# First batch's down projection in rounded high and low parts, two heads later

## The chip, the cores and the metric

One NeuronCore of one Trainium2 chip. The metric is the device time of one execution in microseconds; the median of several executions counts. Before: 638.56 us, median of 3 runs (638.52 to 638.67).

## The reference, cut to what matters

```python
# q, k, v: (2, 8, 768, 64); sliding window of 128 keys plus 4 sink keys; softmax; times v
x = attention(q, k, v)                      # (2, 768, 512)
# mixer 1: U (768, 32), V (32, 768), w_ch1 (512, 2048), w_ch2 (2048, 512)
h = x.transpose(0, 2, 1) @ U @ V            # x.T @ U is the "down projection" of this case
u = x + h.transpose(0, 2, 1)
x = u + np.maximum(u @ w_ch1, 0.0) @ w_ch2
# mixer 2: the same form with w_tok1 (768, 256), a relu, w_tok2, and 1536 hidden channels
```

All in fp32.

## The kernel before

TensorE is faster on a rounded fp32 format (float32r) than on plain fp32. To keep fp32 precision, an operand is cut in a high part (rounded by ScalarE's Copy, L858, L942) and a low part (the operand less its high part, by GpSimd, L837, L543, or VectorE, L1148). A product is then three rounded matmuls (high·high, high·low, low·high), or two where one side carries both of its parts in its columns.

`plan` is one list of steps. Every engine goes through it in order and issues its own instructions for each step, with semaphore waits between engines. An engine's queue is strictly in order: what stands behind a waiting instruction waits as well. The order of the plan is therefore the order of the work.

**Attention, first batch.** Tiles T = 0 to 5 of 128 queries, 8 heads each; a head step has the number u = 8T + h. `attention(b)` (L64) builds for each u a unit: scores(u) (three rounded matmuls, L1364), the product with v of step u-4 (`pv`, L1394), and the transposes of the probabilities of u-2 (`probsT`, L1374). For scores(u) VectorE adds the mask and takes the maximum (L1093, "masked" here), ScalarE takes exp (L908), GpSimd copies the sink probabilities (L791). The transposes land in one of two PSUM banks in turn (banks 4 and 0, which qT, kT and sinksT use as well) and are copied to SBUF by ScalarE for odd u (L917), by VectorE for even u (L1112). In between lie, for the next tile, the transposes of q and k (`qT` at head 0, `kT` at head 2, L1341; copies on ScalarE, L868 and L877), and their high and low parts: VectorE's casts (L1048, L1071), GpSimd's subtractions q_lo (L532) and k_lo in two halves (L543; `ksplit` at head 4, `ksplit_odd` at head 6). At head 4 of tile T+1 comes `sinkpv` of tile T (L1403), after which VectorE writes x_nat, the attention's output for tile T (L1122, L1125). Three single pieces also lie on VectorE: a part of v_sink (L1040, ahead of scores 9 and 14), and V4's cast and subtraction (L1131, L1134) behind x_nat of tile 2.

**Down projection, first batch.** `("down", 1, 0, T-1)` stands at the end of head 5 of tile T (T = 1 to 5); the one of tile 5 stands by itself after the attention. It is one plain fp32 matmul (L1422), which the profile shows as two: stationary U3_sb (three copies of U side by side, 96 columns), moving x_nat (512 columns), accumulated over the six tiles in bank 3. ScalarE and VectorE then make of the three row groups the high and low parts in `low4` (L932, L1138), and the up projection multiplies 96 rows of low4 with 96 rows of V4_sb (L1472, L1538).

**Down projection, second batch.** It uses the rounded format already: `usplit` (L933, L1139) makes U4, whose 128 columns per tile are three copies of U's high part and one of its low part; `x1split` (L937, L1145) makes the high and low parts of x; two rounded matmuls per tile (L1415).

After 80 us the mixers run, with the second batch's attention laid between the matmuls of the first batch's mixer.

The lines around the old down projection:

```python
            if b == 0 and h == 5 and T > 0:
                now.append(("down", 1, b, T - 1))
...
                        pe.wait_ge(x_ready, t + 1)
                        last = mm(m_tile(use)[0:3 * RANK, :], U3_sb[:, t, :], x_nat[:, b, t, :],
                                  start=(t == 0), stop=(t == NQ - 1))
```

Of the kernel before, what the change touches and what calls it, by code (L numbers as in the profile page):

```python
# [5 lines left out]
def attention_then_two_mixers(  # L6
# [26 lines left out]
    f32 = mybir.dt.float32  # L33
# [5 lines left out]
    DM = H * D  # L39
# [24 lines left out]
    def attention(b):  # L64

        lo, hi = b * NQ * H, (b + 1) * NQ * H
        units, late = [], []
        LAG_T, LAG_V = LAGS[b]
        for u in range(lo, hi + LAG_V):
            T, h = divmod(u, H)  # L70
            now, scores, probsT, pv = [], [], [], []
            if u == 0:
                now += [("qT", T), ("kT", T), ("qsplit", T), ("ksplit", T)]
            sinks_after = u - (LAG_T if b else LAG_V)
            sinks = [("sinksT", sinks_after // H)] if lo <= sinks_after < hi and sinks_after % H == H - 1 else []
            if b == 0:
                now, sinks = now + sinks, []
            if u < hi and T + 1 < NTILES:
                if h == 0:
                    now.append(("qT", T + 1))  # L80
                if h == (2, 3)[b]:
                    now += [("kT", T + 1), ("qsplit", T + 1)]
                if h == (4, 5)[b]:
                    now.append(("ksplit", T + 1))
                if h == (6, 7)[b]:
                    now.append(("ksplit_odd", T + 1))
            if u < hi:
                scores.append(("scores", u))
            if lo <= u - LAG_T < hi:
                probsT.append(("probsT", u - LAG_T))  # L90
            if lo <= u - LAG_V:
                pv.append(("pv", u - LAG_V))
            sinkpv = [("sinkpv", (u - LAG_V) // H)] if lo <= u - LAG_V and (u - LAG_V) % H == H - 1 else []
            if b == 0 and u < hi + LAG_V - 1:
                pv, late = late + pv, sinkpv
            else:
                pv = pv + late + sinkpv
            now += scores + pv + probsT + sinks
            if u == hi and b == 0:
                now.append(("ksinks", NQ))  # L100
            if b == 0 and h == 5 and T > 0:
                now.append(("down", 1, b, T - 1))
            units.append(now)
        return units
# [191 lines left out]
    with ExitStack() as ctx:  # L296
        def sb(name, shape, dt=f32):
            return ctx.enter_context(nc.sbuf_tensor(name, shape, dt))

        def sem(name):  # L300
            return ctx.enter_context(nc.semaphore(name))
# [26 lines left out]
        with ExitStack() as early:  # L328
# [22 lines left out]
            probs = eb("probs", [P, 4, NK])  # L351
            probs_T = eb("probs_T", [P, 2, 2 * P])

        b_hi = sb("b_hi", [P, 7, 2, HALF], f32r)
        b_lo = sb("b_lo", [P, 7, 2, HALF], f32r)
        x2_hi, x2_lo = (part[:, 5:7].rearrange("p a k t -> p (a k t)")[:, 0:2 * DM].rearrange("p (t d) -> p t d", t=2)
# [57 lines left out]
        probs_ready = sem("probs_ready")  # L414
        psink_ready = sem("psink_ready")
        tp_ready = sem("tp_ready")
        u_high = sem("u_high")
        u_split = sem("u_split")
        x1_high = sem("x1_high")
# [423 lines left out]
        def _(act):  # L843
# [5 lines left out]
            for s in plan:  # L849
# [78 lines left out]
                    act.wait_ge(probs_ready, H * (T + 1))  # L928
                    nc.scalar.add(sums_eps[:, T % 2, :], sums[:, T % 2, :], 1.0e-9).then_inc(eps_added, 1)
                elif s[0] == "down" and s[1] == 1 and s[3] == NQ - 1:  # L930
                    rows = (4 if s[2] else 3) * RANK
                    high_of((s[:3], 0), rows, low4[0:rows, :], ACT.Copy)  # L932
                elif s[0] == "usplit":  # L933
                    act.wait_ge(x_ready, NTILES)
                    for part, ts in zip(U4_parts, (slice(0, KD), slice(KD, NQ))):
# [80 lines left out]
        def _(dve):  # L1016
# [15 lines left out]
            for s in plan:  # L1032
# [103 lines left out]
                elif s[0] == "down" and s[1] == 1 and s[3] == NQ - 1:  # L1136
                    rows = slice(RANK, 2 * RANK)
                    low_of((s[:3], 0), rows, low4[rows, :], low4[rows, :])  # L1138
                elif s[0] == "usplit":  # L1139
                    dve.wait_ge(U_loaded, 48)  # L1140
                    for n, (part, ts) in enumerate(zip(U4_parts, (slice(0, KD), slice(KD, NQ)))):
# [137 lines left out]
        def _(pe):  # L1279
# [52 lines left out]
            for s in plan:  # L1332
# [72 lines left out]
                elif s[0] == "down" and s[1] == 1:  # L1405
                    _, layer, b, t = s
                    use = (s[:3], 0)
                    if t == 0:
                        pe.wait_ge(U_loaded, 48)
                        m_free(use)  # L1410
                    if b:
                        pe.wait_ge(u_split, 2)
                        pe.wait_ge(x1_split, t + 1)
                        for n, x in enumerate((x2_hi, x2_lo)):
                            last = mm(m_tile(use)[:, :], U4_parts[t // KD][:, t % KD, :], x[:, t % 2, :],  # L1415
                                      start=(t == 0 and n == 0), stop=(t == NQ - 1 and n == 1),
                                      skip_group_check=True)
                        if t < NQ - 1:
                            last.then_inc(down1_done, 1)
                    else:  # L1420
                        pe.wait_ge(x_ready, t + 1)
                        last = mm(m_tile(use)[0:3 * RANK, :], U3_sb[:, t, :], x_nat[:, b, t, :],  # L1422
                                  start=(t == 0), stop=(t == NQ - 1), skip_group_check=True)
# [24 lines left out]
                elif s[0] == "up":  # L1448
# [19 lines left out]
                    for d in parts_of(s):  # L1468
                        rows = slice(d * P, (d + 1) * P)
                        if layer == 1:  # L1470
                            ranks = slice(0, (4 if b else 3) * RANK)
                            last = mm(m_tile((s[:4], d))[:, 0:HALF], low4[ranks, rows], V4_sb[ranks, cols],  # L1472
                                      start=False, stop=True, skip_group_check=True)
                        else:
# [44 lines left out]
                elif s[0] == "mm2":  # L1519
# [10 lines left out]
                    for i in range(TPH):  # L1530
# [3 lines left out]
                        if begins(s):  # L1534
                            m_free(use)
                            if layer == 1:
                                ranks = slice(0, (4 if b else 3) * RANK)
                                mm(m_tile(use)[:, :], V4_sb[ranks, here], low4[ranks, :], start=True, stop=False,  # L1538
                                   skip_group_check=True)
                            else:  # L1540
# [39 lines left out]
```

## Time and profile before

| | before |
|---|---|
| median of 3 runs | 638.56 us |
| profiled execution: time, span | 638.47 us, 636.4 us |
| TensorE busy (matmuls; weight loads) | 619.0 us (97%); 556.3 us (87%) |
| VectorE, ScalarE, GpSimd busy | 360.0, 326.5, 396.8 us |
| granted TensorE clock, mean | 1.00 |
| L1422, the fp32 down projection | 12 records, 24.3 to 76.8 us from the start |
| loads of U | 3, issued from 8.6 to 9.8 us, 2.8 us to landing |
| L1472 (up projection, 96 and 128 rows) | 16 records, 0.336, 0.422 and 0.442 us (min, median, max) |
| first mm1 of the first batch's mixer (L1515) | starts at 80.55 us |

All times inside the execution are microseconds from the start of the span. "Busy" of TensorE is modelled, since matmuls overlap; the distance from one start to the next says more. An engine's "idle before" names what it waited for, as inferred from semaphores.

### The profile page before, as it was taken

What the parts mean: (1) busy time and instruction counts of PE and PEld (TensorE: products, weight loads), DVE (VectorE), ACT (ScalarE), POOL (GpSimd) and SP (SyncE); (2) the same over time, 40 slices, a digit from 0 to 9 for tenths busy, and PEclk for the clock granted to TensorE, in tenths of its full rate; (3) what the DMA queues carried; (4) which work ended last, traced back from release to release, by engine and by line L of the source; (5) the groups of instructions that cost most, each with busy time, mean ns of one, the idle gap of its engine ahead of it and who ended that gap; (6) DMA issues with size and microseconds to landing.
All of it is one profiled execution on the core that took longest, in us unless ns stands there. A gap on an engine that the chain in (4) does not pass through costs nothing.

```text
span 636.4 us, 10351 instructions
## 1 busy us (share of the span) xinstructions
PE 619.0 (97%) x3466; PEld 556.3 (87%) x3466; DVE 360.0 (57%) x757; ACT 326.5 (51%) x728; POOL 396.8 (62%) x420
## 2 busy tenths in 40 slices
PE   8899889999999998999999999999999999999997
PEld 7889778989989997999999988899998888999986
DVE  7776664563654546775665741396577226665411
ACT  5657755545545465754454444545444447454321
POOL 8644656878878684557565654576657446667252
PEclk9999999999999999999999999999999999999999
DMA  8444243543343434322323332432333353421252
GB/s 175 108 95 117 71 127 86 132 117 100 92 125 100 134 88 128 92 91 75 110 82 108 91 109 75 120 110 87 95 90 114 91 145 97 148 83 34 51 155 76
DMA packets 88467, 65.59 MB, mean 103 GB/s; under 512 B 43040, under 2 KB 72480, under 8 KB 88416
## 3 DMA queue, kind: packets, MB, share of 16 engines
q1 hardware_dynamic: 88416, 64.95, 36.6%
q8 instruction: 28, 0.46, 0.3%
q14 instruction: 23, 0.19, 0.1%
HBM read 61.52 MB, written 3.15 MB: 102 GB/s over the span
## 4 chain that ended last, share of the span: by engine, by line
PE 85%; DVE 8%; issue 3%; ACT 2%; POOL 1%; DMA 0%; DVEq 0%; ACTq 0%; POOLq 0%
PE bank L1550 33%; PE bank L1321 23%; PE bank L1515 9%; PE bank L1394 4%; PE bank L1364 3%; PE bank L1479 3%; PE bank L1441 3%; PE bank L1374 2%; PE bank L1341 1%; DVE b_lo L1194 1%; PE bank L1455 1%; DVE masked L1093 1%; PE bank L1422 1%; PE bank L1542 1%; DVE b_lo L1148 1%
## 5 line engine op out<-in xcount | busy, mean ns | idle before, releaser
L837 POOL TENSOR_TENSOR w_lo<-w_raw,w_hi 128x512 fp32r<-128x512 f32 (+1 forms) x158 | 208.7, 1328 | 140.8 <-ACT w_hi L858 140.7
L858 ACT ACTIVATE w_hi<-w_raw 128x512 fp32r<-128x512 f32 (+1 forms) x158 | 96.7, 618 | 54.2 <-PE bank L1550 36.2
L1550 PE MATMUL bank<-w_hi,hid_hi 128*128 128x512 f32 x216 | 86.7, 401 | 0.3 <-DVE hid_lo L1025 0.3
L908 ACT ACTIVATE probs<-masked,neg_max 128x264 f32<-128x264 f32 x96 | 49.5, 516 | 70.7 <-DVE neg_max L1093 70.3
L1550 PE MATMUL bank<-w_hi,hid_lo 128*128 128x512 f32 x216 | 85.0, 394 | 0.0
L1550 PE MATMUL bank<-w_lo,hid_hi 128*128 128x512 f32 x216 | 84.9, 393 | 0.0
L1550 PE MATMUL bank<-w_hi,y_hid 128*128 128x512 f32 x216 | 71.0, 394 | 0.2
L1093 DVE CUSTOM_DVE_ANT_0 masked<-bank,masks 128x264 f32<-128x264 f32 x96 | 41.1, 429 | 26.8 <-PE bank L1364 23.3
L1394 PE MATMUL bank<-v_nat,probs_T 128*128 128x64 f32 x352 | 50.7, 263 | 1.8 <-DVE probs_T L1112 1.2
L1394 PEld LDWEIGHTS bank<-v_nat,probs_T 128*128 128x128 f32 x352 | 48.0, 190 | 3.8 <-ACT probs_T L917 1.7
L1550 PEld LDWEIGHTS bank<-w_hi,y_hid 128*128 128x128 f32 x216 | 40.5, 188 | 9.5 <-POOL w_lo L837 1.5
L1550 PEld LDWEIGHTS bank<-w_hi,hid_lo 128*128 128x128 f32 x216 | 40.5, 188 | 8.9
L1321 PE MATMUL bank<-b_hi,a_hi_even 128*128 128x384 f32 x140 | 47.1, 336 | 0.1
L1550 PEld LDWEIGHTS bank<-w_hi,hid_hi 128*128 128x128 f32 x216 | 40.7, 188 | 7.4 <-issue 0.7
L1321 PE MATMUL bank<-b_hi,a_lo_even 128*128 128x384 f32 x140 | 47.0, 336 | 0.0
L1321 PE MATMUL bank<-b_hi,a_lo_odd 128*128 128x384 f32 x140 | 47.0, 336 | 0.0
L1321 PE MATMUL bank<-b_hi,a_hi_odd 128*128 128x384 f32 x140 | 46.9, 335 | 0.0
L1321 PE MATMUL bank<-b_lo,a_hi_odd 128*128 128x384 f32 x140 | 46.9, 335 | 0.0
L1321 PE MATMUL bank<-b_lo,a_hi_even 128*128 128x384 f32 x140 | 46.9, 335 | 0.0
L1550 PEld LDWEIGHTS bank<-w_lo,hid_hi 128*128 128x128 f32 x216 | 40.6, 188 | 6.7
L1515 PE MATMUL bank<-uT_hi,w_hi 128*128 128x384 f32 x128 | 45.3, 354 | 0.4 <-DVE uT_lo L1028 0.4
L1025 DVE SCALAR_TENSOR_TENSOR hid_lo<-bank,hid_hi 128x384 fp32r<-128x384 f32 x32 | 17.8, 556 | 48.4 <-ACT hid_hi L846 48.4
(173 smaller groups left out, 1528.7 us busy)
## 6 DMA issues: line engine op xcount, KB each, us to landing
w_raw<-in_moe_w_ch_dram SPq DMA_DIRECT2D x144, 256.0 KB, 2.7
w_raw<-in_moe_w_ch_dram SPq DMA_DIRECT2D x20, 512.0 KB, 3.5
q_nat<-in_q_dram SPq DMA_DIRECT2D x12, 256.0 KB, 3.0
k_nat<-in_k_dram SPq DMA_DIRECT2D x12, 256.0 KB, 3.5
v_nat<-in_v_dram SPq DMA_DIRECT2D x12, 256.0 KB, 3.5
out_dram<-o_stage SPq DMA_DIRECT2D x11, 256.0 KB, 3.4
w_raw<-in_moe_w_tok_dram SPq DMA_DIRECT2D x6, 256.0 KB, 2.6
w_raw<-in_moe_w_tok_dram SPq DMA_DIRECT2D x8, 192.0 KB, 2.4
```

The lines of the kernel that those rows point to most:

```text
L837: nc.gpsimd.tensor_tensor(w_lo[:, split % NW, 0:n], w_raw[:, split % NR, 0:n], w_hi[:, split % NW, 0:n].bitcast(f32), ALU.subtract) \
L858: nc.scalar.activation(w_hi[:, split % NW, 0:n], w_raw[:, split % NR, 0:n], ACT.Copy) \
L908: nc.scalar.activation(probs[:, u % 4, :], masked[:, u % 3, :], ACT.Exp, bias=neg_max[:, u % (2 * H):u % (2 * H) + 1], scale=-1.0, accum_o ...
L1025: nc.vector.scalar_tensor_tensor(out=dst, in0=src, scalar=0.0, in1=hi.bitcast(f32), op0=ALU.max, op1=ALU.subtract).then_inc(m_drained, 1)
L1093: nc.vector.tensor_tensor_reduce(out=masked[:, u % 3, :], in0=s_slots(u)[0][:, 0:NK], in1=masks[:, mask_of(T), :], scale=1.0, scalar=3.0e3 ...
L1321: last = mm(bank[:, 0:HALF], w[at % 2][:, a, k, :], u[:, b_part, k, :], start=(first and n == 0), stop=(n == 5), skip_group_check=True)
L1364: last = mm(bank[:, 0:NK], queries, keys(ks, T, h // 2, h % 2), start=(n == 0), stop=(n == len(passes) - 1))
L1394: last = mm(o_bank(T)[:, h * D:(h + 1) * D], probs_T[:, u % 2, j * P:(j + 1) * P], v_nat[:, tile % 3, h * D:(h + 1) * D], start=(h == 0 an ...
L1441: last = mm(m_tile(use)[:, :], w[:, slot, cols], x[:, t % 2, :], start=(t == 0 and n == 0), stop=(t == NQ - 1 and n == 2), skip_group_chec ...
L1479: last = mm(m_tile((s[:4], d))[:, 0:HALF], tok[:, g, rows], w[:, slot, 0:HALF], start=False, stop=(g == KG - 1 and n == 2), skip_group_che ...
L1515: last = mm(m_tile(use)[:, 0:HALF], w[:, slot, rows], u[:, kk, cols], start=(n == 0), stop=(n == 3 * KD - 1))
L1550: last = mm(m_tile(use)[:, :], stationary, w[:, slot, :], start=False, stop=(final and n == 2), skip_group_check=True)
```

## The change

In the first batch the down projections of tiles 0 to 4 are made as in the second batch: a step `u0split` (end of head 1 of tile 1) makes U4 for all six tiles in an unused part of uT_lo, 128 x 576 columns on ScalarE and 128 x 192 on VectorE. A step `x0split` (end of head 5 of tile T) makes the high and low parts of x of tile T-1, 128 x 512 each, in two slots in uT_hi and uT_lo. The down projection itself moves from the end of head 5 to the end of head 7 and waits for both steps. Tile 5 stays one fp32 matmul in its old place, into 96 of the 128 rows. low4 and V4_sb are used with 128 rows in both batches.

```diff
--- before.py
+++ after.py
@@ -98,7 +98,11 @@
             now += scores + pv + probsT + sinks
             if u == hi and b == 0:
                 now.append(("ksinks", NQ))
+            if u == H + 1:
+                now.append(("u0split",))
             if b == 0 and h == 5 and T > 0:
+                now.append(("x0split", T - 1))
+            if b == 0 and h == 7 and T > 0:
                 now.append(("down", 1, b, T - 1))
             units.append(now)
         return units
@@ -350,6 +354,9 @@
             masked = eb("masked", [P, 3, NK])
             probs = eb("probs", [P, 4, NK])
             probs_T = eb("probs_T", [P, 2, 2 * P])
+
+        x0_hi, x0_lo = (part[:, 0:2, 0:DM] for part in (uT_hi, uT_lo))
+        U4_first = uT_lo[:, KD - 1, :].rearrange("p (t r) -> p t r", t=NQ)
 
         b_hi = sb("b_hi", [P, 7, 2, HALF], f32r)
         b_lo = sb("b_lo", [P, 7, 2, HALF], f32r)
@@ -414,6 +421,11 @@
         probs_ready = sem("probs_ready")
         psink_ready = sem("psink_ready")
         tp_ready = sem("tp_ready")
+        u0_high = sem("u0_high")
+        u0_split = sem("u0_split")
+        x0_high = sem("x0_high")
+        x0_split = sem("x0_split")
+        down0_done = sem("down0_done")
         u_high = sem("u_high")
         u_split = sem("u_split")
         x1_high = sem("x1_high")
@@ -928,8 +940,16 @@
                     act.wait_ge(probs_ready, H * (T + 1))
                     nc.scalar.add(sums_eps[:, T % 2, :], sums[:, T % 2, :], 1.0e-9).then_inc(eps_added, 1)
                 elif s[0] == "down" and s[1] == 1 and s[3] == NQ - 1:
-                    rows = (4 if s[2] else 3) * RANK
-                    high_of((s[:3], 0), rows, low4[0:rows, :], ACT.Copy)
+                    high_of((s[:3], 0), 4 * RANK, low4[:, :], ACT.Copy)
+                elif s[0] == "u0split":
+                    act.wait_ge(U_loaded, 48)
+                    nc.scalar.activation(U4_first[:, :, 0:3 * RANK], U3_sb[:, :, :], ACT.Copy).then_inc(u0_high, 1)
+                elif s[0] == "x0split":
+                    t = s[1]
+                    act.wait_ge(x_ready, t + 1)
+                    if t >= 2:
+                        act.wait_ge(down0_done, t - 1)
+                    nc.scalar.activation(x0_hi[:, t % 2, :], x_nat[:, 0, t, :], ACT.Copy).then_inc(x0_high, 1)
                 elif s[0] == "usplit":
                     act.wait_ge(x_ready, NTILES)
                     for part, ts in zip(U4_parts, (slice(0, KD), slice(KD, NQ))):
@@ -1136,6 +1156,16 @@
                 elif s[0] == "down" and s[1] == 1 and s[3] == NQ - 1:
                     rows = slice(RANK, 2 * RANK)
                     low_of((s[:3], 0), rows, low4[rows, :], low4[rows, :])
+                elif s[0] == "u0split":
+                    dve.wait_ge(U_loaded, 48)
+                    dve.wait_ge(u0_high, 1)
+                    nc.vector.tensor_tensor(U4_first[:, :, 3 * RANK:4 * RANK], U3_sb[:, :, 0:RANK],
+                                            U4_first[:, :, 0:RANK].bitcast(f32), ALU.subtract).then_inc(u0_split, 1)
+                elif s[0] == "x0split":
+                    t = s[1]
+                    dve.wait_ge(x0_high, t + 1)
+                    nc.vector.tensor_tensor(x0_lo[:, t % 2, :], x_nat[:, 0, t, :], x0_hi[:, t % 2, :].bitcast(f32),
+                                            ALU.subtract).then_inc(x0_split, 1)
                 elif s[0] == "usplit":
                     dve.wait_ge(U_loaded, 48)
                     for n, (part, ts) in enumerate(zip(U4_parts, (slice(0, KD), slice(KD, NQ)))):
@@ -1408,7 +1438,14 @@
                     if t == 0:
                         pe.wait_ge(U_loaded, 48)
                         m_free(use)
-                    if b:
+                    if b == 0 and t < NQ - 1:
+                        pe.wait_ge(u0_split, 1)
+                        pe.wait_ge(x0_split, t + 1)
+                        for n, x in enumerate((x0_hi, x0_lo)):
+                            last = mm(m_tile(use)[:, :], U4_first[:, t, :], x[:, t % 2, :],
+                                      start=(t == 0 and n == 0), stop=False, skip_group_check=True)
+                        last.then_inc(down0_done, 1)
+                    elif b:
                         pe.wait_ge(u_split, 2)
                         pe.wait_ge(x1_split, t + 1)
                         for n, x in enumerate((x2_hi, x2_lo)):
@@ -1468,7 +1505,7 @@
                     for d in parts_of(s):
                         rows = slice(d * P, (d + 1) * P)
                         if layer == 1:
-                            ranks = slice(0, (4 if b else 3) * RANK)
+                            ranks = slice(0, 4 * RANK)
                             last = mm(m_tile((s[:4], d))[:, 0:HALF], low4[ranks, rows], V4_sb[ranks, cols],
                                       start=False, stop=True, skip_group_check=True)
                         else:
@@ -1534,7 +1571,7 @@
                         if begins(s):
                             m_free(use)
                             if layer == 1:
-                                ranks = slice(0, (4 if b else 3) * RANK)
+                                ranks = slice(0, 4 * RANK)
                                 mm(m_tile(use)[:, :], V4_sb[ranks, here], low4[ranks, :], start=True, stop=False,
                                    skip_group_check=True)
                             else:
```

## Rows read from the trace of the kernel before

**Rows 1.** Windows: stretch, its length, busy us (instructions) of PE, PEld, DVE, ACT, POOL, clock, DMA.
```profile
14.00:20.00 6.00, 4.62 (x34) 4.03 (x34) 4.87 (x20) 4.28 (x17) 3.82 (x8) 1.00 0.69 157
...
29.00:39.00 10.00, 9.86 (x82) 8.89 (x81) 6.71 (x25) 6.84 (x24) 5.33 (x11) 1.00 0.35 80
```

**Rows 2.** Line L1422: min/median/max ns of one, first and last start; idle before it.
```profile
L1422 PE MATMUL bank<-x_nat,U_sb x12: 592/616/670, 24.3 to 76.8; 128*96 128x512 f32 x12
...
  DVE x_nat L1125: 3.9, 8
```

**Rows 3.** Timeline, tile 2, heads 4 to 7: start us, duration us, engine, line.
```profile
33.63 0.29 PE L1364 MATMUL bank<-k_lo,q_hi 128*128 128x264 f32 x1
...
34.98 0.42 DVE L1093 CUSTOM_DVE_ANT_0 masked<-bank,masks 128x264 f32<-128x264 f32 x1
...
35.45 0.52 ACT L908 ACTIVATE probs<-masked,neg_max 128x264 f32<-128x264 f32 x1 [0.91 <-DVE neg_max L1093]
...
35.85 0.29 PE L1364 MATMUL bank<-k_lo,q_hi 128*128 128x264 f32 x1
...
35.97 0.36 ACT L917 ACTIVATE probs_T<-bank 128x256 f32<-128x256 f32 x1
...
36.29 0.43 DVE L1093 CUSTOM_DVE_ANT_0 masked<-bank,masks 128x264 f32<-128x264 f32 x1 [0.88 <-PE bank L1364]
36.45 1.28 POOL L543 TENSOR_TENSOR k_lo<-uT_full,k_hi 64x512 fp32r<-64x512 f32 x1
...
36.84 0.28 PE L1364 MATMUL bank<-k_lo,q_hi 128*128 128x264 f32 x1
...
38.89 0.39 PE L1374 MATMUL bank<-ident,probs 128*128 128x128 f32 x2
```

**Rows 4.** Timeline of TensorE at the second batch's down projection, a rounded pair.
```profile
243.46 0.39 PE L1415 MATMUL bank<-b_hi 128*128 128x512 f32 x1
...
243.91 0.39 PE L1415 MATMUL bank<-b_hi 128*128 128x512 f32 x1
```

**Rows 5.** Lines of the second batch's splits: min/median/max ns of one.
```profile
L942 ACT ACTIVATE b_hi<-x_nat x6: 614/625/633, 236.9 to 244.7; 128x512 fp32r<-128x512 f32 x6
...
L1148 DVE TENSOR_TENSOR b_lo<-x_nat,b_hi x6: 676/688/1776, 238.3 to 246.2; 128x512 fp32r<-128x512 f32 x6
...
L936 ACT ACTIVATE b_hi<-U_sb x1: 514/514/514, 236.2 to 236.2; 128x384 fp32r<-128x384 f32 x1
L936 ACT ACTIVATE b_lo<-U_sb x1: 353/353/353, 236.6 to 236.6; 128x192 fp32r<-128x192 f32 x1
...
L1143 DVE TENSOR_TENSOR b_lo<-U_sb,b_lo x1: 209/209/209, 238.2 to 238.2; 128x64 fp32r<-128x64 f32 x1
```

**Rows 6.** A GpSimd subtraction in the timeline, and line L1083, which began beside it.
```profile
72.67 1.27 POOL L837 TENSOR_TENSOR w_lo<-w_raw,w_hi 128x512 fp32r<-128x512 f32 x1 [0.62 <-ACT w_hi L858]
...
L1083 DVE TENSOR_TENSOR k_lo<-uT_full,k_hi x2: 206/752/1298, 72.7 to 74.0; 64x48 fp32r<-64x48 f32 x2
```

**Rows 7.** Timeline, tile 3, the same places: k_lo, and transposes of step 30.
```profile
48.80 1.28 POOL L543 TENSOR_TENSOR k_lo<-uT_full,k_hi 64x512 fp32r<-64x512 f32 x1
...
50.65 0.39 PE L1374 MATMUL bank<-ident,probs 128*128 128x128 f32 x2
```

**Rows 8.** Timeline, tile 1 (u0split's place, then x0split's), and tile 5.
```profile
19.96 0.58 ACT L877 ACTIVATE uT_full<-bank 128x512 f32<-128x512 f32 x1
...
20.44 0.51 ACT L908 ACTIVATE probs<-masked,neg_max 128x264 f32<-128x264 f32 x1
...
26.25 1.28 POOL L543 TENSOR_TENSOR k_lo<-uT_full,k_hi 64x512 fp32r<-64x512 f32 x1
...
28.39 0.39 PE L1374 MATMUL bank<-ident,probs 128*128 128x128 f32 x2
...
69.88 1.29 POOL L543 TENSOR_TENSOR k_lo<-uT_full,k_hi 64x512 fp32r<-64x512 f32 x1
...
72.12 0.66 PE L1394 MATMUL bank<-v_nat,probs_T 128*128 128x64 f32 x4 [0.21 <-ACT probs_T L917]
```

## Prediction, made before the changed kernel was run

> **What bounds the kernel now.** I read the busy shares and the windows first, then the costliest lines, then the waits, and last the timeline around each place that is edited. Over the whole span TensorE is busy 97%, and from 80 us on, in the mixers, nearly without a gap. The change lies before that, in the first batch's attention (about 9 to 77 us). There the windows show TensorE 9.86 of 10 us busy beside VectorE 6.71 and ScalarE 6.84 [rows 1]. That looks like a stage paced by TensorE, and by it the change would be a gain. The timeline says less. A head step u (scores, probs·V of u-4, transposes of u-2) goes round a ring of three engines: scores on TensorE, masked on VectorE (L1093), exp on ScalarE (L908), transposes on TensorE, their copy on ScalarE (odd u) or VectorE (even u), product on TensorE. Each engine takes its part in the order of the plan. The ring has some 1.5 us of slack, and the down projection sits where it is smallest: in head 5 of each query tile VectorE has just made x_nat (0.69 us), so its copy of step u-3's transposes and masked(u) are late, and TensorE waits 3.9 us in all for x_nat before L1422 [rows 2]. From one key-low scores matmul to the next the step with the down projection takes 33.63 to 35.85 = 2.22 us, the ordinary one after it 35.85 to 36.84 = 0.99 [rows 3]: the fp32 down costs 1.23 us, some 0.93 of it work (two passes of the array of 0.616 us as recorded, overlapping; the next instruction is through 0.93 us after) and 0.3 waiting.
>
> **TensorE's part: less work.** Five times an fp32 pair (0.93 us) becomes two rounded matmuls of 128x512. The second batch already does the same; a pair there takes 243.46 to 243.91 = 0.45 us [rows 4]. That is 0.48 us less, 2.4 us over five tiles. Moved from head 5 to head 7 it no longer waits for x_nat. The last tile stays fp32 and stays where it was (0). The matmuls with V4 and low4 take 128 rows in place of 96, and a matmul's time goes by its columns: in both forms L1472 is 0.34 to 0.44 us, so 0. ScalarE's reading of the down bank has 128 partitions in place of 96, 512 columns as before: 0.
>
> **What is added.** ScalarE: x high, 128x512, five times 0.625 us; U high, 576 columns, once. Its two neighbours are 0.514 us for 384 columns and 0.353 for 192, so 0.84 ns a column and 0.675 us. VectorE: x low, 0.688 us when undisturbed, five times; U low, 192 columns, between 0.209 (64 columns) and 0.688 (512), near the small one: 0.35 us [rows 5]. Together 3.8 us on each, in 70 us of which each is 60 to 70% busy. By shares both fit. They are charged by place.
>
> **x0split, head 5 of query tile 2 (u = 21).** It stands behind the end of step 21, so ScalarE does exp(21), the copy of step 19's transposes, and only then x high; VectorE does masked(21) and then *stands* before x low until x high is there, with masked(22), the copy of step 20 and masked(23) queued behind it. In the old timeline exp(21) starts at 35.45 and the copy at 35.97 [rows 3]; neither depends on the removed matmul, since both hang on VectorE's x_nat and masked(21) at 34.98. So x high runs about 36.3 to 36.9. VectorE, free from 35.4, starts x low near 36.9, where before masked(22) had started at 36.29.
> Then GpSimd. At 36.45 it starts its k_lo subtraction (1.28 us, to 37.73), and that start hangs on exp(21) and does not move. x low reads two SBUF operands, as k_lo does. Where such a VectorE operation meets a GpSimd one in this trace, it ends with it: L1083, 64x48, took 1298 ns beside a GpSimd subtraction from 72.67 to 73.94 and 206 ns after it [rows 6]; L1148's longest of six is 1776 ns against a median of 688 [rows 5]. I therefore let x low end at 37.73 + 0.56 = 38.29 (its own columns, about 0.68 less the start-up that passes while it waits), not at 37.6.
> The Trainium skill has this as a rule ("SBUF — State Buffer", "SBUF: two separate sides"): the port pair shared by VectorE and GpSimd is an exclusive lock, taken for a whole instruction by a VectorE op with two SBUF inputs or by a GpSimd op. By it x low waits in all five tiles; the trace agrees at L1083. By the same skill's "VectorE: DVE Perf Modes" alone, which puts an fp32 two-input operation of 512 columns at 691 ns, it would be through in 0.69 us: that is the second case below.
> From there the chain is: masked(22) 0.36, copy of 20's transposes 0.33 (both start to start, since neighbouring VectorE rows overlap by some 0.08), masked(23) 0.43, exp(23) 0.52, ScalarE's copy of 21's transposes 0.36 (its PSUM bank is the one that the transposes of 22 need), and two hops between engines of 0.04, less the 0.08 by which masked(22) overlaps x low: 2.0 us. Transposes(22) start at 40.29, where they stood at 38.89 [rows 3]: **+1.4 us**. The down pair itself waits for x low (38.3, TensorE arrives at 36.9) and lies inside this; so the 0.48 us saved per pair, and the removed wait, buy an earlier arrival at a longer wait. Afterwards the ring runs as before and the next x_nat is as late as the ring, so nothing is given back before the next tile.
>
> **The other tiles, by the same steps:** end of k_lo, + 0.56, + 2.0, against the old start of the matching TensorE work.
> Tile 4 repeats tile 2: +1.4.
> Tile 3: k_lo 48.80 + 1.28; 52.64 against 50.65 [rows 7]: +2.0. Here VectorE's V4 cast and subtraction had delayed everything already, and the old down projection lay hidden behind them; taking it away gains nothing here.
> Tile 1: k_lo 26.25 + 1.28; here the v_sink subtraction (L1040, as many columns as x low: 0.6 us start to start) also queues behind x low; 30.7 against 28.39 is 2.3 [rows 8]; GpSimd's earlier work might start it 0.3 earlier: I take +2.1.
> Tile 5: k_lo 69.88 + 1.29; 73.73 against 72.12 [rows 8]: +1.6, passed on through scores(48) to the last x_nat and so to the first up projection.
>
> **u0split, head 1 of tile 1.** ScalarE's 0.675 us goes ahead of the k copy that started at 19.96; VectorE stands for it, does U low, and only then q_hi's cast and masked(10), which it had long done. 19.96 + 0.67 + 0.04 + 0.27 + 0.34 + 0.43 + 0.04 = 21.75 for exp(10), against 20.44 [rows 8]: +1.3, of which about **+1.2** reaches x_nat of tile 0. The chip shows in this stretch no slack on TensorE that would help, since it waits there for these very engines. Bounds: 0.6 (ScalarE's part alone counts) to 1.9. U has landed by 12.6 us, so no wait for it.
>
> **Sum.** 1.2 + 2.1 + 1.4 + 2.0 + 1.4 + 1.6 = +9.7 us. After 80 us the mixers run on a busy TensorE, with the same work in the same order, so nothing is absorbed and nothing is added. The profiled execution took 638.47 us (span 636.4), 0.09 below the median of 638.56. Forecast 648.2.
> Bounds: each x0split is 0.7 less without the meeting with GpSimd, or about 0.3 more if the k copy and exp of the next tile come late on ScalarE as well; u0split 0.6 to 1.9. So +5.6 to +11.9.
>
> **The rivals.**
> 1. *The queues hold, the meeting on SBUF does not count* (x low slips in before k_lo, or both run): five times 0.7 less, +6.1, 644.6. For it: five of L1148's six were at most a little over a median of 0.69. Against: those lie where GpSimd was idle. 0.17.
> 2. *TensorE paces the stage* (other side). The place is the same five steps, the price 2.22 - 0.99 - 0.45 = 0.78 us gained in tiles 2, 3 and 4, and by the same difference 1.1 and 1.5 in tiles 1 and 5, -4.9 us: 633.6. It decides if exp(22) is done before TensorE comes to transposes(22), then at 38.89 - 0.78 = 38.1; so masked(22) would have to start before 37.1, within 0.8 us of its old 36.29. I get 38.2. For it: TensorE 9.86 of 10. 0.07.
> 3. *The slack swallows it*: two units between scores and transposes absorb what is added, the gain and the loss cancel: within 0.2%. 0.03.
> 4. *The clock*. In every stretch shown the granted clock is 1.00, its upper level (2.4 GHz), and TensorE held it even where it was busy 4.62 of 6 us [rows 1]. New idle stretches are at most 1.5 us each. If it fell to 1.2 GHz for a few us at tile 1 or 3, 3 us and more would be added: 651 to 654. 0.05.
> That the change does not do what it says (the matmuls stay slow) costs nothing extra, as the pairs wait anyway; it is within the likeliest.
>
> **How the numbers follow.** Likeliest case 0.68, with 645.5 to 650.5 of its own. The range takes in it and rival 1, and the upper bound of the sum: 642.5 to 651. About what a measurement of this kernel can tell from no change is 0.2%, 1.3 us. Slower 0.90 (likeliest, rivals 1 and 4), same 0.03, faster 0.07.
>
> **What would show it.** Right: x low at about 1.4 us in five rows, each ending some 0.56 us after a GpSimd k_lo; TensorE waiting at the new down pair for VectorE's x low; ScalarE idle before exp(22) some 2 us; the tile period (between L1125 rows) 1.2 to 2 us longer; the first mm1 of the mixer near 90 us in place of 80.5; the rest of the span unchanged in length. Wrong: masked of head 6 within 0.5 us of its old place behind masked of head 5, x low at 0.69 us, or a first mm1 before 85 us.

## The result and the profile after

The changed kernel takes 654.35 us (650.63 to 655.33, 4 runs) against 638.62 us: 1.0232 times the time before, 95% interval 1.0216 to 1.0248. It is slower, as forecast, but by 15.7 us where 9.7 were forecast, and outside the range. The profiled run took 653.6 us. On the page, the span has grown by 15.5 us, TensorE is less busy by share, and the granted clock, all 9s before, has two lower digits (7 and 6):

```profile
span 651.9 us, 10371 instructions
...
PE 626.9 (96%) x3466; PEld 561.9 (86%) x3466; DVE 366.6 (56%) x763; ACT 330.0 (51%) x734; POOL 396.8 (61%) x420
...
PEclk9997969999999999999999999999999999999999
```

The work added by the split is where it was expected. The x low parts, by line (min/median/max ns, then what VectorE waited for, then who waited):

```profile
L1167 DVE TENSOR_TENSOR uT_lo<-x_nat,uT_hi x5: 1381/1386/1387, 27.6 to 80.7; 128x512 fp32r<-128x512 f32 x5
its engine sat idle before it (us, times) until:
  ACT uT_hi L952: 7.3, 5
who waited for it (us, times):
  PE bank L1445: 5.1, 5
```

They take 1.39 us each, twice the undisturbed 0.688 [rows 5], all five. U low, with its one wait:

```profile
L1162 DVE TENSOR_TENSOR uT_lo<-U_sb,uT_lo x1: 357/357/357, 20.5 to 20.5; 128x192 fp32r<-128x192 f32 x1
its engine sat idle before it (us, times) until:
  ACT uT_lo L946: 1.5, 1
```

The timeline of tile 2 answers to [rows 3], 3.5 us later since tile 1 has already lost that much:

```profile
38.97 0.52 ACT L920 ACTIVATE probs<-masked,neg_max 128x264 f32<-128x264 f32 x1 [0.91 <-DVE neg_max L1113]
...
39.48 0.36 ACT L929 ACTIVATE probs_T<-bank 128x256 f32<-128x256 f32 x1
...
39.74 0.62 ACT L952 ACTIVATE uT_hi<-x_nat 128x512 fp32r<-128x512 f32 x1
...
39.96 1.27 POOL L555 TENSOR_TENSOR k_lo<-uT_full,k_hi 64x512 fp32r<-64x512 f32 x1
...
40.40 1.39 DVE L1167 TENSOR_TENSOR uT_lo<-x_nat,uT_hi 128x512 fp32r<-128x512 f32 x1 [1.46 <-ACT uT_hi L952]
41.70 0.42 DVE L1113 CUSTOM_DVE_ANT_0 masked<-bank,masks 128x264 f32<-128x264 f32 x1
...
41.93 0.47 PE L1445 MATMUL bank<-uT_hi,uT_lo 128*128 128x512 f32 x1 [1.15 <-DVE uT_lo L1167]
...
43.87 0.41 PE L1404 MATMUL bank<-ident,probs 128*128 128x128 f32 x2
```

ScalarE's exp(21), its copy and x high follow one another (38.97, 39.48, 39.74); VectorE waits 1.46 us and starts x low at 40.40, beside GpSimd's k_lo, which runs from 39.96 to 41.23; x low ends at 41.79, 0.56 us after it. masked(22) starts at 41.70, where it would have been at 39.81 by the old distance from exp(21) (36.29 - 35.45). The new down pair (L1445) starts after a wait of 1.15 us, and transposes(22) at 43.87, 4.90 us after exp(21) in place of 3.44.

The starts of x_nat, one row of the timeline for each tile, date the loss:

| x_nat of tile | before | after | added since the last | forecast |
|---|---|---|---|---|
| 0 (u0split before it) | 23.48 | 24.75 | 1.27 | 1.2 |
| 1 (x0split in tile 1) | 34.05 | 37.56 | 2.24 | 2.1 |
| 2 | 44.53 | 49.56 | 1.52 | 1.4 |
| 3 | 56.30 | 65.24 | 3.91 | 2.0 |
| 4 | 67.48 | 77.90 | 1.48 | 1.4 |
| 5 | 75.59 | 89.28 | 3.27 | 1.6 |
| end of span | 636.4 | 651.9 | 1.81 | 0 |

Four steps come out within 0.15 us. The other three are 1.9, 1.7 and 1.8 us over, and they are the stretches in which the clock was down (windows, columns as in [rows 1]; the clock is the number after the five busy times):

```profile
46.00:50.00 4.00, 4.00 (x37) 3.77 (x37) 3.35 (x12) 2.85 (x11) 2.47 (x5) 1.00 0.80 183
50.00:54.00 4.00, 2.09 (x15) 1.58 (x14) 2.71 (x6) 1.22 (x5) 1.24 (x4) 0.93 0.06 14
54.00:58.00 4.00, 3.51 (x14) 2.80 (x15) 2.42 (x6) 1.78 (x7) 1.50 (x3) 0.50 0.00 0
...
84.00:88.00 4.00, 3.88 (x20) 3.89 (x20) 2.19 (x6) 1.93 (x7) 1.32 (x2) 0.52 0.18 62
88.00:92.00 4.00, 3.80 (x10) 1.85 (x9) 1.69 (x6) 2.33 (x6) 1.60 (x3) 0.50 0.01 3
```

Between 54 and 58 us and again around 84 to 92 TensorE was granted 0.50, its lower level of 1.2 GHz. In windows of 1 us there are two falls: one from about 53.4 to 60.2, in tile 3, and one from about 84.1 to 94.4, which covers the end of the attention and the start of what follows it. The same scores matmul takes 0.37 us before and 0.57 after the fall:

```profile
52.39 0.66 PE L1424 MATMUL bank<-v_nat,probs_T 128*128 128x64 f32 x4 [1.86 <-DVE probs_T L1132]
...
53.03 0.37 PE L1394 MATMUL bank<-k_hi,q_hi 128*128 128x264 f32 x1
...
57.49 0.57 PE L1394 MATMUL bank<-k_hi,q_hi 128*128 128x264 f32 x1
```

Ahead of the first fall TensorE had waited 1.86 us for VectorE's copy of the transposes (it was behind V4's work), and was busy only 2.09 of 4 us from 50 to 54. The first matmul of the mixer starts 15.45 us later than before (80.55; the forecast was near 90), and the distance from there to the end is unchanged:

```profile
96.00 0.41 PE L1552 MATMUL bank<-uT_hi,w_hi 128*128 128x384 f32 x1 [0.39 <-DVE uT_lo L1048]
```

### The profile page after: what moved, and what is told of

Read it like the earlier page. It is cut to its first block, busy times and chain, and to the rows that moved or that the text cites. A ratio compares the mean times of both kernels' runs of the same rounds, so it can differ in the third digit from the quotient of the medians.

```text
span 651.9 us, 10371 instructions
## 1 busy us (share of the span) xinstructions
PE 626.9 (96%) x3466; PEld 561.9 (86%) x3466; DVE 366.6 (56%) x763; ACT 330.0 (51%) x734; POOL 396.8 (61%) x420
## 4 chain that ended last, share of the span: by engine, by line
PE 83%; DVE 7%; ACT 2%; issue 2%; POOL 1%; DVEq 0%; ACTq 0%
PE bank L1587 32%; PE bank L1351 22%; PE bank L1552 8%; PE bank L1424 4%; PE bank L1394 3%; PE bank L1516 3%; PE bank L1478 3%; PE bank L1404 2%; PE bank L1492 2%; DVE b_lo L1224 1%; PE bank L1371 1%; PE bank L1579 1%; DVE b_lo L1178 1%; POOL w_lo L849 1%; DVE uT_lo L1167 1%
## 5 line engine op out<-in xcount | busy, mean ns | idle before, releaser
L1424 PE MATMUL bank<-v_nat,probs_T 128*128 128x64 f32 x352 | 53.8, 273 | 4.5 <-DVE probs_T L1132 3.5
L1424 PEld LDWEIGHTS bank<-v_nat,probs_T 128*128 128x128 f32 x352 | 50.2, 198 | 8.6 <-DVE probs_T L1132 5.3
L803 POOL COPY p_sink<-probs 128x12 f32<-128x12 f32 x96 | 20.1, 212 | 43.1 <-ACT probs L920 40.1
```

What stands on the lines that cost most here:

```text
L803: nc.gpsimd.tensor_copy(p_sink[:, T % 2, :].rearrange("p (c n) -> p c n", c=3)[:, :, N_SINK * h:N_SINK * (h + 1)], probs[:, u % 4, P:BLK]. ...
L1424: last = mm(o_bank(T)[:, h * D:(h + 1) * D], probs_T[:, u % 2, j * P:(j + 1) * P], v_nat[:, tile % 3, h * D:(h + 1) * D], start=(h == 0 an ...
```

## The experiments

My theory after the result had two terms: about 9.8 us lost in the queues' order (as forecast), and some 5.5 us because the new idle time of TensorE let its clock fall. Its rivals: the clock explains everything and the delays alone would be absorbed; ScalarE and VectorE are too full for the splits wherever they lie; TensorE's new wait, not the split, is what costs. Each time is compared with the kernel before on the same chip. Three chips were used: one for e1, e2, e3 and v1, a second for e4, e5 and e8, a third for e9, v2, v3 and v4. The kernel before kept a mean clock of 0.999 or more in all of its 43 runs on them.

### u0split alone (e1)

```diff
+            if u == H + 1:
+                now.append(("u0split",))      # U4 is made and not used
             if b == 0 and h == 5 and T > 0:
                 now.append(("down", 1, b, T - 1))
```

> The kernel before with u0split alone (U4 is made and not used). Queue theory: ScalarE's 0.68 us and VectorE's wait and 0.36 us stand in the way of q_hi's cast and masked(10), and x_nat of tile 0 comes 1.2 to 1.3 us later, as in the changed kernel (23.48 to 24.75): 639.8, clock 1.00. Rival, the loss is the clock's alone and such delays are absorbed: 638.6.

Measured: 640.03 us against 638.67, ratio 1.0022 (1.0013 to 1.0030). x_nat of tile 0 starts at 24.99 in place of 23.48, and of tile 5 at 77.11 in place of 75.59: 1.5 us are lost at once and none comes back, as the queue theory says. The result is a little above the 1.3 expected. Four of its eleven runs also had a mean clock of 0.997 (640.03 to 641.23 us; the seven at 1.000 took 639.65 to 640.21), which was not expected. Those four have no trace. In the profiled run, at 1.00, TensorE's longest wait between 12 and 96 us is 0.77 us, where it was 0.79 before, so where the clock fell in the others is open.

### The move alone (e2), and the move with TensorE kept busy (e9)

```diff
-            if b == 0 and h == 5 and T > 0:
+            if b == 0 and h == 7 and T > 0:      # e2 and e9; the matmul stays plain fp32
                 now.append(("down", 1, b, T - 1))
...
+    FILL = {30: 14}                             # e9 only
...
+                    for _ in range(FILL.get(u, 0)):
+                        mm(bank[:, 0:NK], high, keys(k_hi, T, h // 2, h % 2), start=True, stop=True)
```

> The kernel before with the five fp32 down projections at head 7 in place of head 5, nothing else. Queue theory: the waits for x_nat go (0.3 us in tiles 2 and 4, some 0.6 in tile 1, 1.0 in tile 5), while in tile 3 the 0.93 us of work comes out from behind V4's work (+0.6): -1.6 us, 637.0. Rival, the move itself makes TensorE idle and the clock fall: slower than 640 with a clock under 1.

> e2 (the fp32 down projections at head 7) with the first pass of scores(30) repeated 14 times, 1.55 us of work in the 1.9 us for which TensorE waited in tile 3 behind VectorE's V4 work. If e2's clock fell for that idle stretch: clock 1.00 everywhere and the 637.0 that the queues gave e2 (below the kernel before). If the fall has another cause: 641 as e2.

Measured: e2 641.47 against 638.67, ratio 1.0042 (1.0030 to 1.0055), clock 0.997 in four runs of five; the fifth had 1.000 and took 639.86. e9 639.92 against 638.89, ratio 1.0013 (1.0004 to 1.0023), clock 1.00 (once 0.999) in eleven runs. In tile 3 of e2 the timeline shows what the old down projection had covered:

```profile
45.54 0.28 PE L1364 MATMUL bank<-k_hi,q_both 128*128 128x264 f32 x1
46.23 0.95 DVE L1134 TENSOR_TENSOR V_sb<-o_stage,V_sb 32x768 fp32r<-32x768 f32 x1
47.21 0.42 DVE L1112 COPY probs_T<-bank 128x256 f32<-128x256 f32 x1
...
47.69 0.81 PE L1394 MATMUL bank<-v_nat,probs_T 128*128 128x64 f32 x4 [1.86 <-DVE probs_T L1112]
...
48.57 0.57 PE L1364 MATMUL bank<-k_hi,q_hi 128*128 128x264 f32 x1
```

V4's subtraction holds VectorE until 47.2, TensorE waits 1.86 us, and 0.9 us later its matmuls are slow (0.57 for a scores matmul). Before, the down projection stood in this wait and left 0.61 us of it:

```profile
45.28 1.10 PE L1422 MATMUL bank<-x_nat,U_sb 128*96 128x512 f32 x2
...
47.35 0.66 PE L1394 MATMUL bank<-v_nat,probs_T 128*128 128x64 f32 x4 [0.61 <-DVE probs_T L1112]
```

With 1.55 us of repeated matmuls in that gap (e9) the clock stays up, and the time equals that of e2's one run in which it did not fall. By e2's own runs such a fall costs 1.3 to 2.9 us. This speaks for the idle time as the cause, but e2 and e9 ran on different chips, and no run repeats e2 on e9's chip; the comparison on one chip is e5.

Both theories missed e9's level: without the clock the move costs 1.0 us, where I expected it to save 1.6. From x_nat to x_nat tiles 1 to 5 of e9 change by +0.19, +0.27, +0.85, +0.25 and -0.35 us. The 0.85 lies in tile 3, where +0.6 was expected for the matmul that comes out from behind V4's work. The repeated matmuls can hardly be in it, since e2's run without a fall takes the same time. In the other tiles the saving came in tile 5 alone, and there 0.35 of 1.0. The reason stands in tile 2 of e2:

```profile
33.70 0.29 PE L1364 MATMUL bank<-k_lo,q_hi 128*128 128x264 f32 x1
...
34.72 0.41 DVE L1112 COPY probs_T<-bank 128x256 f32<-128x256 f32 x1
...
35.19 0.66 PE L1394 MATMUL bank<-v_nat,probs_T 128*128 128x64 f32 x4
...
37.16 1.02 PE L1422 MATMUL bank<-x_nat,U_sb 128*96 128x512 f32 x2
...
38.02 0.60 PE L1341 MATMUL bank<-ident,q_nat 128*128 128x128 f32 x4
```

The q transposes of the kernel before:

```profile
37.69 0.60 PE L1341 MATMUL bank<-ident,q_nat 128*128 128x128 f32 x4
```

From one key-low matmul (33.70) to the q transposes (38.02) it takes 4.32 us, against 33.63 to 37.69 = 4.06 before. The wait for x_nat is gone, but TensorE reaches the next product sooner and waits there for VectorE's copy (34.72), which x_nat delays all the same.

### The splits alone (e3), and the same waits with fp32 (e8)

```diff
# e3: x0split and u0split as in the change, results unused
             if b == 0 and h == 5 and T > 0:
-                now.append(("x0split", T - 1))
-            if b == 0 and h == 7 and T > 0:
-                now.append(("down", 1, b, T - 1))
+                now += [("x0split", T - 1), ("down", 1, b, T - 1)]
# e3 and e8: the matmul and the 96 rows of low4 as before; e8 keeps the change's place and waits, e3 waits for x_nat
-                        for n, x in enumerate((x0_hi, x0_lo)):
-                            last = mm(m_tile(use)[:, :], U4_first[:, t, :], x[:, t % 2, :], ...
+                        last = mm(m_tile(use)[0:3 * RANK, :], U3_sb[:, t, :], x_nat[:, b, t, :], ...
```

> The kernel before with u0split and x0split added and their results unused; the down projection stays plain fp32 at head 5 and waits for x_nat alone. Queue theory: nearly the whole loss is here without any change of TensorE's work, since masked of head 6 is late all the same: x_nat of tile 2 near 37.5, +9 to +10 us without the clock (648), up to 654 if the clock falls too. Rival, the loss comes from TensorE waiting at the new down projection: under +3 (641).

> The changed kernel with its waits and splits, but the five down projections as one plain fp32 matmul each (0.93 us for 0.46). Queue theory: TensorE waits for VectorE there, so the 0.47 us are mostly hidden, 0 to 0.25 us a tile: 0 to +1.3 us against the changed kernel, perhaps less clock lost: 650 to 655. Rival, TensorE paces the stage: the full 2.4 us more, 656.

Measured: e3 653.01 against 638.67, ratio 1.0232 (1.0207 to 1.0256); e8 653.02 against 638.45, ratio 1.0236 (1.0203 to 1.0270). Both equal the changed kernel within their intervals. The splits alone make the whole loss, although TensorE never waits for them in e3; it waits elsewhere (waits of TensorE up to 96 us, total, times, longest):

```profile
PE bank L1370 <- DVE probs_T L1131: 6.4, 4, 2.0
PE bank L1423 <- DVE probs_T L1131: 2.3, 3, 1.2
PE bank L1442 <- DVE x_nat L1144: 1.6, 4, 0.7
```

The clock was down in both (means of 0.978 to 0.995). In e3 the old down projection still stands at head 5, and TensorE's clock falls all the same, behind waits for the copy of the transposes in tile 1 and in tile 3:

```profile
31.28 0.86 PE L1370 MATMUL bank<-ident,q_nat 128*128 128x128 f32 x4 [2.02 <-DVE probs_T L1131]
...
58.68 0.94 PE L1370 MATMUL bank<-ident,q_nat 128*128 128x128 f32 x4 [1.84 <-DVE probs_T L1131]
```

Behind the same waits in tiles 2 and 4 (1.26 and 1.25 us) it stays at 1.00.

Halving the matmul's work where TensorE waits for VectorE anyway (the change against e8) is worth nothing that can be measured in the total, where the clock varies by more. From x_nat to x_nat, in the tiles in which the clock was up in both, it is worth 0.00, 0.10 and 0.14 us (tiles 1, 2 and 4: 12.81, 12.00, 12.66 against 12.81, 12.10, 12.80) of the 0.47 us of work.

### x low without GpSimd beside it (e4)

```diff
-                if h == (6, 7)[b]:
+                if h == 7:
                     now.append(("ksplit_odd", T + 1))
```

> The changed kernel with the second half of k_lo (GpSimd) one head later, at head 7. If x low's 1.39 us are half waiting for GpSimd: L1167 at 0.69 us, each tile 0.7 us shorter, -3.5 us against the changed kernel, and less idle TensorE, so the clock may fall for less long: 645 to 650. If x low is slow for its own sake: L1167 stays at 1.39 us and the time at 653.

Measured: 649.16 against 638.45, ratio 1.0170 (1.0140 to 1.0199). x low now takes its bare time:

```profile
L1167 DVE TENSOR_TENSOR uT_lo<-x_nat,uT_hi x5: 691/691/693, 27.8 to 79.1; 128x512 fp32r<-128x512 f32 x5
```

So the second 0.7 us of each x low were the meeting with k_lo. (The rule of the Trainium skill that the prediction used, "SBUF — State Buffer", "SBUF: two separate sides", agrees with the trace of the changed kernel in all five tiles.) But tiles 2 and 4 shrink only by 0.25 and 0.21 us, not by the 0.7 expected (11.75 and 12.45 from x_nat to x_nat, after 12.00 and 12.66): the q transposes start 0.68 us earlier than in the changed kernel, and then k_lo, put later, holds up scores(25):

```profile
41.93 0.63 PE L1371 MATMUL bank<-ident,q_nat 128*128 128x128 f32 x4
...
42.48 1.27 POOL L555 TENSOR_TENSOR k_lo<-uT_full,k_hi 64x512 fp32r<-64x512 f32 x1
...
43.80 0.39 PE L1394 MATMUL bank<-k_hi,q_hi 128*128 128x264 f32 x1 [0.21 <-POOL k_lo L555]
```

Most of the 4 to 5 us gained come with the clock, which was 0.988 to 0.997, against 0.983 to 0.992: in the profiled run of e4 it fell in tile 3 only.

### The changed kernel with TensorE kept busy (e5)

```diff
+    FILL = {8 * T + h: 5 for T in range(1, 6) for h in (6, 7)}
+    FILL.update({30: 14, 31: 8, 47: 8})
...
+                    if u in FILL:
+                        for _ in range(FILL[u]):
+                            mm(bank[:, 0:NK], high, keys(k_hi, T, h // 2, h % 2), start=True, stop=True)
```

> The changed kernel with the first pass of scores repeated 5 times at heads 6 and 7 of each tile (14 and 8 times at steps 30 and 31, 8 at step 47), each written over by the next, so that TensorE works where it stood idle. If the clock fell because TensorE was idle there: clock 1.00 in all stretches and 648 to 649.5, the loss that the queues alone explain, though TensorE has 10 us more work. If the clock does not go by TensorE's idleness, or the queues cost nothing: 653 or more.

Measured: 649.16 against 638.45, ratio 1.0163 (1.0146 to 1.0180), although TensorE issues 65 more matmuls. Two of the four runs had a mean clock of 1.000 and took 648.24 and 648.29; the other two 0.997 and 650.0 and 650.3. In the windows where the changed kernel was slow (same columns) the clock is up:

```profile
50.00:54.00 4.00, 4.00 (x36) 3.96 (x36) 3.89 (x10) 1.48 (x5) 1.89 (x3) 1.00 0.64 145
54.00:58.00 4.00, 3.27 (x27) 2.84 (x26) 2.47 (x6) 1.40 (x4) 1.47 (x2) 1.00 0.00 0
...
84.00:88.00 4.00, 3.24 (x24) 2.67 (x24) 3.17 (x10) 3.13 (x11) 1.46 (x2) 1.00 0.10 33
88.00:92.00 4.00, 3.64 (x22) 2.64 (x21) 1.53 (x4) 3.01 (x9) 2.73 (x4) 1.00 0.26 84
```

From x_nat to x_nat tiles 3 and 5 now take 13.88 and 9.57 us, that is 2.1 and 1.5 more than before (forecast 2.0 and 1.6); tiles 2 and 4 are as in the changed kernel, so the repeated matmuls cost nothing there. On the same chip none of the eight runs of e4 and e8 reached a mean of 1.000; two of the four of e5 did. In those two the change loses 9.8 us, and 9.7 were forecast.

But the clock was not at 1.00 in all stretches, as the idle-time theory had it. The profiled run is one of the two at 0.997: in tile 1 the mean clock was 0.66 from 30 to 34 us, behind two waits of only 0.72 and 0.82 us, although heads 6 and 7 had their five repeated matmuls each. The q transposes there are already slow:

```profile
31.27 1.09 PE L1373 MATMUL bank<-ident,q_nat 128*128 128x128 f32 x4 [0.82 <-DVE probs_T L1134]
```

The changed kernel had waits of 1.15 and 0.82 us in the same place and kept 1.00. So filling the gaps of tiles 3 and 5 kept the clock up there, but the length of one wait does not decide by itself whether it falls.

### The splits where the engines are idle (v1, v3, v2, v4)

```diff
# v1 (x high ahead of exp of head 5; low parts on GpSimd; down pair one tile later)
+            if b == 0 and h == 5 and 0 < T < NQ:
+                now.append(("x0high", T - 1))
             now += scores + pv + probsT + sinks
+            if u == 3:
+                now.append(("u0high",))
...
+            if b == 0 and h == 6 and 0 < T < NQ:
+                now.append(("x0low", T - 1))          # v4: h == 7, on VectorE
+            if b == 0 and (h == 1 and 1 < T < NQ or u == hi + 2):   # v3, v2, v4: h == 3
+                now.append(("down", 1, b, T - 2 if u < hi else NQ - 2))
# v3 = v1 with U low at u = 8, down pair at head 3, FILL = {30: 14}
# v2 = v3 without FILL, V4's cast on ScalarE and its low part on GpSimd:
+            if b == 0 and u in (3 * H + 6, 4 * H + 3):
+                now.append(("V4high",) if u == 3 * H + 6 else ("V4low",))
```

> The change laid where the engines are idle: U high on ScalarE after the copy of step 1's transposes, x high on ScalarE ahead of exp of head 5 (where it waited 0.9 us), both low parts on GpSimd after k_lo's second half, the rounded down pair at head 1 of the next tile (that of tile 4 before the last). Queue theory: nothing stands in the ring's way, the pairs save 2.4 us and most waits for x_nat go, less up to 1 us for GpSimd meeting VectorE's casts: -2 to -4, 635 to 636.5, clock 1.00. Rival, ScalarE and VectorE and GpSimd are simply too full for the splits wherever they lie: over 640.

> v1 with the down pair at head 3 in place of head 1, U low at step 8, and the same 14 repeated passes at step 30. Queue theory and clock: v1 less its 1.7 us of clock, 0.8 us of waiting for GpSimd: 637 to 638. If what keeps v1 above the kernel before is GpSimd's load: 640 or more, clock 1.00.

> v3 without repeated passes, but with V4's cast on ScalarE (head 6 of tile 3) and its low part on GpSimd (head 3 of tile 4), so that VectorE does not hold the ring in tile 3. That wait was 1.9 us and the fall of the clock behind it 1.7: 635 to 636.5, clock 1.00, the fastest of all. If the ring loses elsewhere what it gains here: 638 and more.

> v2 with x low back on VectorE, but at the end of head 7, where VectorE waited 1.1 us for TensorE and GpSimd's k_lo is over. If the place and not VectorE's load made the change slow: within 1 us of v2 (635 to 637), L of x low at 0.69 us. If VectorE has no room for x low anywhere: some 0.7 us a tile more than v2, 639.

| | time | before | ratio (95%) | clock |
|---|---|---|---|---|
| v1 | 640.65 | 638.67 | 1.0031 (1.0021 to 1.0040) | 0.997, once 1.000 (639.44 us) |
| v3 | 636.85 | 638.89 | 0.9967 (0.9955 to 0.9980) | 1.000 |
| v2 | 635.41 | 638.89 | 0.9944 (0.9932 to 0.9957) | 1.000 |
| v4 | 635.87 | 638.89 | 0.9953 (0.9941 to 0.9966) | 0.999 to 1.000 |

v1 missed, and its rival "over 640" gave the time. Like e2 it uncovers V4's work in tile 3 (a wait of 1.99 us, with the clock down behind it), and its down pair waited for GpSimd's U low (0.5 us). The clock is not all: its one run at 1.000 still took 0.8 us more than the kernel before, where 2 to 4 less were expected. v3 moves the pair and U low and fills the gap: tiles 1 and 2 become 1.2 and 0.5 us shorter than in v1, and the kernel is 2.0 us faster than before. v2 takes V4's work out of VectorE's way and is the fastest, 3.5 us under the kernel before. Part of v2's and v4's gain is then not the change's: V4's work was moved as well, and the kernel before with that move alone was not run. v3 is the measure of the splits and the rounded pair at a better place.

In v2's tile 2 x high (L976) starts after x_nat and is done at 34.58, as masked(21) is, so exp(21) at 34.63 does not wait for it, and x low lies on GpSimd behind k_lo:

```profile
33.95 0.63 ACT L976 ACTIVATE uT_hi<-x_nat 128x512 fp32r<-128x512 f32 x1 [0.23 <-DVE x_nat L1169]
...
34.63 0.52 ACT L941 ACTIVATE probs<-masked,neg_max 128x264 f32<-128x264 f32 x1
...
37.13 1.29 POOL L846 TENSOR_TENSOR uT_lo<-x_nat,uT_hi 128x512 fp32r<-128x512 f32 x1
```

v4, with x low on VectorE again, two heads later than the change had it, is 0.5 us behind v2. I expected x low there to be clear of k_lo, at 0.69 us. It was not: in four of the five tiles it met k_lo's second half again and was about as long as in the changed kernel.

```profile
L1174 DVE TENSOR_TENSOR uT_lo<-x_nat,uT_hi x5: 687/1419/1540, 26.9 to 67.8; 128x512 fp32r<-128x512 f32 x5
```

So VectorE has room for x low, even at 1.4 us a time, where less hangs on what stands behind it: the places of the splits made the change slow, and not the meeting by itself. But v4 differs from the change in more than x low's place: x high lies ahead of exp, U low and V4's low part stay on GpSimd, V4's cast on ScalarE, and the down pair one tile later. Which of these is worth how much was not taken apart.

## Why the prediction was right and wrong

- *ScalarE and VectorE fit by shares, but not by place*: right. The stretch from exp(21) to transposes(22) grew by 1.46 us for a forecast 1.4, and e3 shows that the splits alone do it.
- *x low waits for GpSimd's k_lo*: right, 1381 to 1387 ns in five tiles, ending 0.55 to 0.56 us after it. Its worth to the total was mis-sized in the rival (0.7 a tile); with k_lo moved e4 found 0.21 to 0.25. e4 puts k_lo on the ring's path, so what the meeting costs by itself in this place is not measured; in v4 four such meetings go with a kernel 0.5 us behind v2.
- *TensorE's saving and the removed wait buy nothing*: right but for 0.1 us a tile for the saving (change against e8). The rival "TensorE paces the stage" (-4.9 us) fell. That removing the wait for x_nat would bring 0.3 us a tile even in the move alone was wrong (e2, e9): it comes back as a wait for the copy.
- *u0split +1.2*: 1.27 in the changed kernel, 1.5 alone, and 1.9 in e3, e5 and e8, with the same code for this step; why it varies is open. *Tiles 1, 2, 4*: 2.24, 1.52 and 1.48 for 2.1, 1.4 and 1.4. *Tiles 3 and 5*: 2.1 and 1.5 with the clock up (e5) for 2.0 and 1.6. The terms as the traces show them with the clock up add up to 10.0 us, or 10.6 with the larger u0split. That two runs of e5 gave 9.8 for 9.7 is a closer agreement than the terms have, and partly luck.
- *The step that failed* is rival 4, "The clock": "New idle stretches are at most 1.5 us each", and with it "After 80 us ... nothing is added". I had worked out when VectorE and ScalarE come late, but had not drawn TensorE's own idle time from it. In tile 3 the old down projection (45.28 to 46.2) filled most of TensorE's wait behind V4's work; I wrote that taking it away "gains nothing here", and did not see that it leaves 1.86 us idle, with 0.49 us more at the new down pair. TensorE's clock fell there and again at the end of tile 5, and that cost 1.9 + 1.7 + 1.8 = 5.4 us: the clock's term in the sum was nothing and should have been this. The removed matmul is not needed for it. In e3 it stays, and the delays by the splits alone reach TensorE as single waits of up to 2.02 us; each of my delays was added to the time, but none was followed to TensorE as an idle stretch. That the clock had held at 4.62 of 6 us busy [rows 1] was no bound for 2.09 of 4. e5 shows the cause in tiles 3 and 5, and e9, on another chip than e2, in tile 3: with TensorE busy in those gaps the clock stays up there.
- The chance given to that case was 0.05 and its time 651 to 654; the measured median, 654.35, lies just above. The range ended below it.

Why the second fall comes just where it does stays open: it follows waits of 0.66, 1.15 and 0.37 us in tile 5, while tile 4 has a wait of 1.14 and no fall, and e8's profiled run has waits of 0.67 and 1.15 at the same place of tile 5 and no fall either. How much of a run is slow also changes from run to run (clock 0.983 to 0.992 in the changed kernel).

## What to carry to other kernels

Charge work added to an in-order queue by what stands behind it at that place, not by the engine's share: the same splits and the same rounded pair cost 15 us in one place (9.8 with the clock up) and gained 2.0 in another (v3). When a matmul is removed or moved, or another engine is delayed, ask how long TensorE will stand idle in one stretch; its clock may fall there, which cost 5.4 us here on top of the delays. Before a step is placed, look for the row in which each engine waits, and for what GpSimd runs beside it.

## What the runs showed of the hardware

- TensorE's clock fell in the profiled run of e2 behind one idle stretch of 1.86 us with TensorE busy before it, and four of e2's five runs had the same mean, 0.997; with 14 matmuls put in the gap, on another chip, none of eleven fell under 0.999. It also fell behind waits of 0.72 and 0.82 us (e5, tile 1), and held behind waits of 1.14 to 1.26 us (tiles 2 and 4 of the changed kernel and e3). The Trainium skill ("TensorE: Matmul & The Clock Gate", Part 1) says that activity is what releases the throttle; e2 with e9, and tiles 3 and 5 of e5, agree.
- A VectorE subtraction of 512 columns with two SBUF operands, begun 0.29 to 0.48 us after a GpSimd one, ends 0.54 to 0.56 us after it: 1381 to 1387 ns in five tiles of the changed kernel, 1.34 to 1.54 us in four tiles of v4, in place of 691.
- Two rounded 128x512 matmuls in place of one plain fp32 one: 0.45 us for 0.93, and 0.00 to 0.14 us a tile in time where TensorE waits for another engine (e8).
